# Reordered loads, scans and products and another cut of the last tile in a three-stage attention, channel-mix and convolution kernel

## The chip, the cores and the metric
One core of one Trainium2 chip. The metric is the time of one execution on the device in microseconds, as the median of several runs. TensorE (PE in the rows) multiplies, with its weight loads shown apart (PEld); VectorE (DVE), ScalarE (ACT) and GpSimd (POOL) do elementwise work; SP issues DMA transfers in the order of its program.

## The reference
Three layers follow each other, on 2 sequences of 768 positions with 8 heads of 64 features (512 in all).

```python
# 1: decayed linear attention, block by block (lam near 0.98 for each head)
intra = einsum('bhic,bhjc->bhij', qb, kb) * Dmask          # lam ** (i - j) for i >= j
out   = einsum('bhij,bhjd->bhid', intra, vb) + einsum('bhid,bhde->bhie', qb * lam_pow, kv_state)
kv_state = lam_block * kv_state + einsum('bhsd,bhse->bhde', kb * rev_pow, vb)
# 2: channel mix
xk = mu_k * x + (1 - mu_k) * x_prev ;  xr = mu_r * x + (1 - mu_r) * x_prev
k = maximum(xk @ w_k, 0) ;  v = k * k @ w_v ;  x = sigmoid(xr @ w_r) * v      # w_k 512x1024, w_v 1024x512
# 3: gated projection
gate = sigmoid(causal convolution of x with 5 taps per channel)
out = (gate * (x @ w_val)) @ w_out
```

## The kernel before
**Attention** runs over 12 chunks of 128 positions (6 for each sequence), heads in four pairs. For each chunk n, TensorE does `scores(n)` (keys against queries, fp32, into PSUM), `inter(n)` (state against the decayed queries qd), `attend(n)` (values against the weighted scores pT) and `update(n)` (values against the decayed keys kdec). VectorE does `weigh(n)`, scores times the decay matrix dec, and `new_state(n)`. GpSimd does `decay_k(n)` and `decay_q(n)`, which give kdec and qd. ScalarE does `fade(n)` (the state times one decay) and `evacuate_x(p)`, which copies the sums of a pair of chunks out of PSUM into x as soon as both are attended. Each engine has one list of work, written out by hand; a wait in it holds all that stands behind it. The order of TensorE is in lines 851 to 900, that of the others at the ends of their blocks.

**Decays.** dec (8 scans, line 592) and qdec (4 scans, line 598) are made on VectorE from `prm`, a 20 KB table that also holds the mixing and convolution parameters. ScalarE's queue loads prm (line 414); SP's queue loads all else, in the order of lines 225 to 246: qk (queries and keys, 512 KB a chunk) and kv (keys and values by position, 512 KB, or 256 KB where a chunk has no update), then w_k, w_r and w_v in pieces of 1024 columns. Eight input buffers; a load into a used one waits for the products that read it.

**Channel mix and projection** run over 3 tiles of 512 positions, with the features on partitions. A product with a weight is done in three passes of fp32r matmuls (`three_pass`, lines 692 to 698): high x high, low x high, high x low, where `high` is a rounded copy (ScalarE) and `low` the remainder (`low` on GpSimd, line 289, or on VectorE, line 537). `hidden(t, n)` is one of 8 products of 12 matmuls with w_k, `receptance(t, m)` one of 4 with w_r, `value(t, m)` one of 4 products of 24 matmuls with w_v. Piece i of w_k serves hidden n = 2i and 2i+1. ScalarE's `relu` and VectorE's `square` take each hidden result out of PSUM, `kk_high` and `kk_low` split it, and `value(t, 0)` waits for all eight low parts. `mix_part` (ScalarE), `mix` (VectorE), `mix_high` and `mix_low` make xk and xr from x; the ones for xr of tile 0 need x of attention's last pair, so `evacuate_x(5)`.

**The end.** `project(t, c)` gives 128 positions of output, `evacuate` copies them (line 406), SP stores them (line 257). The last one is done in two halves of 256 columns, each with its own copy (line 411) and store (line 262), so that the first half is stored while the second is multiplied.

Of the kernel before, what the change touches and what calls it, by code (L numbers as in the profile page):

```python
# [31 lines left out]
WARM = 8  # L32
PIECE = 1024
OUT_CH = NT * CT


LAM_A, LAM_B, MU, CONV = 0, H, H + PAIRS, H + PAIRS + 2 * KT
# [12 lines left out]
def build(nc, prm_in, qk_in, kv_in, w_k, w_v, w_r, w_val, w_out, out):  # L50
    with ExitStack() as ctx:
        def sem(name):
            return ctx.enter_context(nc.semaphore(name))
# [8 lines left out]
        def place(name, shape, at, dt=F32):  # L62
# [82 lines left out]
            sem(z) for z in "p_ready state_ready kdec_ready qd_ready faded_ready x_ready".split()]  # L145
        wk_hi, wk_lo, wr_hi, wr_lo, wv_hi, wv_lo, w2_hi, w2_lo = [
            sem(z) for z in "wk_hi wk_lo wr_hi wr_lo wv_hi wv_lo w2_hi w2_lo".split()]
        wk_lo_first = sem("wk_lo_first")
        (xk_part, xk_full, xk_hi, xk_lo, xr_part, xr_full, xr_hi, xr_lo) = [
            sem(z) for z in "xk_part xk_full xk_hi xk_lo xr_part xr_full xr_hi xr_lo".split()]  # L150
        h_done, r_done, v_done, val_done, proj_done = [
# [53 lines left out]
        @block.sync  # L205
        def _(sp):
            def free(n):

                if n >= IN_BUFS:
                    sp.wait_ge(att_done, n - IN_BUFS + 1)  # L210
                    sp.wait_ge(update_done, updates(n - IN_BUFS))

            def load_qk(n):
                free(n)
                sp.dma_start(qk[n % IN_BUFS][:, :, :], qk_in[n]).then_inc(qk_here[n % IN_BUFS], 16)

            def load_kv(n):
                free(n)
                first = 0 if has_update(n) else 1
                sp.dma_start(kv[n % IN_BUFS][:, first:, :], kv_in[n, :, first:, :]).then_inc(kv_here[n % IN_BUFS], 16)  # L220

            def load_weight(raw, src, i, done):
                sp.dma_start(raw[:, i * PIECE:(i + 1) * PIECE], src[:, i * PIECE:(i + 1) * PIECE]).then_inc(done[i], 16)

            load_qk(0)
            load_qk(1)
            load_kv(0)
            load_kv(1)
            for p in range(1, NP - 1):
                load_qk(2 * p)  # L230
                load_qk(2 * p + 1)
                load_kv(2 * p)
                load_kv(2 * p + 1)
            load_qk(NCH - 2)
            load_qk(NCH - 1)
            load_weight(wk_raw, w_k, 0, wk_here)
            load_kv(NCH - 2)
            load_kv(NCH - 1)
            for i in range(1, 4):
                load_weight(wk_raw, w_k, i, wk_here)  # L240
            for i in range(2):
                load_weight(wr_raw, w_r, i, wr_here)
            sp.wait_ge(att_done, IN_BUFS)
            sp.wait_ge(update_done, updates(IN_BUFS - 1))
            for i in range(4):
                load_weight(wv_raw, w_v, i, wv_here)

            sp.wait_ge(h_done, FT * NT)
            for i in range(4):
                src = w_val if i < 2 else w_out  # L250
                sp.dma_start(w2_raw[:, i * PIECE:(i + 1) * PIECE],
                             src[:, i % 2 * PIECE:(i % 2 + 1) * PIECE]).then_inc(w2_here[i], 16)

            for n in range(OUT_CH):
                if n < OUT_CH - 1:
                    sp.wait_ge(out_ready, n + 1)
                    sp.dma_start(out[n * CH:(n + 1) * CH, :], out_sb[n // CT][:, n % CT, :]).then_inc(stored, 16)
                else:
                    for half in range(2):
                        cols = slice(half * DM // 2, (half + 1) * DM // 2)  # L260
                        sp.wait_ge(out_ready, n + 1 + half)
                        sp.dma_start(out[n * CH:(n + 1) * CH, cols], out_sb[n // CT][:, n % CT, cols]).then_inc(stored, 16)
            sp.wait_ge(stored, 16 * (OUT_CH + 1))

        @block.gpsimd
        def _(pool):
# [30 lines left out]
                                    pattern=[[-1, P]], channel_multiplier=1).then_inc(ident_ok, 1)  # L297
            pool.wait_ge(dec_ok, H)
            decay_k(0)
            decay_k(1)  # L300
            pool.wait_ge(qdec_ok, PAIRS)
            decay_q(1)
            decay_q(2)
            decay_k(2)
            decay_k(3)
            decay_q(3)
            for p in range(2, NP):
# [1 line left out]
                decay_k(2 * p + 1)  # L309
                decay_q(2 * p)  # L310
                decay_q(2 * p + 1)
            for i in range(1, 4):
                low(wk, wk_raw, i, wk_hi, wk_lo)
            for i in range(2):
                low(wr, wr_raw, i, wr_hi, wr_lo)
# [4 lines left out]
        def _(act):  # L320
# [81 lines left out]
            def evacuate(t, c):  # L402
                n = CT * t + c
                if n < OUT_CH - 1:
                    act.wait_ge(proj_done, n + 1)
                    nc.scalar.copy(out_sb[t][:, c, :], ps[:, bank_of("proj", t, c), :]).then_inc(out_ready, 1)
                else:
                    for half in range(2):
                        cols = slice(half * DM // 2, (half + 1) * DM // 2)
                        act.wait_ge(proj_done, n + 1 + half)  # L410
                        nc.scalar.copy(out_sb[t][:, c, cols],  # L411
                                       ps[:, (bank_of("proj", t, c) + half) % 8, 0:DM // 2]).then_inc(out_ready, 1)

            act.dma_start(prm[:, :], prm_in).then_inc(prm_here, 16)
            act.wait_ge(warm_ok, 1)
            nc.scalar.activation(spare[:, :], warm[:, 0:1], ACT.Sigmoid)
            act.wait_ge(qdec_ok, PAIRS)
# [11 lines left out]
                mix_high(0, k, 0)  # L429
            fade(8)  # L430
            evacuate_x(3)
            fade(9)
            mix_high(0, 3, 0)
            fade(10)
            evacuate_x(4)
            for i in range(3):
                high(wk, wk_raw, i, wk_here, wk_hi)
            evacuate_x(5)
            high(wk, wk_raw, 3, wk_here, wk_hi)
# [58 lines left out]
        def _(dve):  # L498
# [93 lines left out]
                nc.vector.tensor_tensor_scan(dec[:, i, :], prm[:, LAM_A + i:LAM_A + i + 1].to_broadcast([P, CH]),  # L592
                                             ident[:, :], 0.0, ALU.mult, ALU.add).then_inc(dec_ok, 1)
            dve.wait_ge(dec_ok, H)
            weigh(0)
            dve.wait_ge(zero_ok, 1)
            for a in range(PAIRS):
                nc.vector.tensor_tensor_scan(qdec[:, a, :], prm[:, LAM_B + a:LAM_B + a + 1].to_broadcast([P, CH]),  # L598
                                             zeros[:, :], 1.0, ALU.mult, ALU.add).then_inc(qdec_ok, 1)
            nc.vector.tensor_scalar(om[:, :], prm[:, MU:MU + 2 * KT], -1.0, 1.0, ALU.mult, ALU.add).then_inc(om_ok, 1)  # L600

            dve.wait_ge(halo_ok, B)
# [10 lines left out]
            for p in range(2, NP):  # L613
                new_state(2 * p)
                if p + 1 < NP:
                    weigh(2 * p + 2)
                    weigh(2 * p + 3)
                new_state(2 * p + 1)
                if p == 2:
                    mix(0, 0, 0)  # L620
                    mix(0, 1, 0)
                    mix(0, 2, 0)
                if p == 3:
                    mix(0, 3, 0)
                    mix_low(0, 0, 0)
                    mix_low(0, 1, 0)
                if p == 4:
                    mix_low(0, 2, 0)
                    mix_low(0, 3, 0)
                if p == 5:  # L630
                    low(wk, wk_raw, 0, wk_hi, wk_lo_first)
            for k in range(KT):
                mix(0, k, 1)

# [54 lines left out]

        @block.tensor  # L690
        def _(pe):
            def three_pass(to, pairs):
                last = len(pairs) - 1
                for i, (left, right) in enumerate(pairs):
                    nc.tensor.matmul(to, left(0), right(0), start=(i == 0), stop=False)  # L695
                    nc.tensor.matmul(to, left(0), right(1), start=False, stop=False)  # L696
                    done = nc.tensor.matmul(to, left(1), right(0), start=False, stop=(i == last))  # L697
                return done
# [74 lines left out]
            def hidden(t, n):  # L773
                if n == 0:
                    pe.wait_ge(xk_lo, KT * (t + 1))
                    if t == 0:
                        pe.wait_ge(p_ready, 2 * NCH)
                if t == 0 and n == 0:
                    pe.wait_ge(wk_lo_first, 1)
                elif t == 0 and n % 2 == 0:  # L780
                    pe.wait_ge(wk_lo, n // 2)
                if t == 0 and n == 2:
                    pe.wait_ge(x_ready, NP - 1)
                if t == 0 and n == 4:
# [20 lines left out]
            def value(t, m):  # L805
                if m == 0:
                    pe.wait_ge(kk_lo, FT * (t + 1))
                    pe.wait_ge(wv_lo, 4)
                pe.wait_ge(sq_ready, FT * t + KT + m + 1)
                three_pass(ps[:, bank_of("mlp", t, FT + KT + m), :],  # L810
                           [(lambda z, f=f: wv[z][:, f * DM + m * P:f * DM + (m + 1) * P], lambda z, f=f: kk[z][:, f, :])
                            for f in range(FT)]).then_inc(v_done, 1)

            def val(t, m):
                if m == 0:
# [13 lines left out]
            def project(t, c):  # L829
# [10 lines left out]
                bank = bank_of("proj", t, c)  # L840
                halves = [(bank, 0, DM)]
                if CT * t + c == OUT_CH - 1:
                    halves = [(bank, 0, DM // 2), ((bank + 1) % 8, DM // 2, DM)]
                    pe.wait_ge(out_ready, CT + 1)
                for b, lo, hi in halves:
                    three_pass(ps[:, b, 0:hi - lo],
# [9 lines left out]
            attend(0)  # L856
            update(0)
            scores(2)
            update(1)
            inter(1)  # L860
            attend(1)
            scores(3)
            inter(2)
            attend(2)
# [7 lines left out]
            for p in range(2, NP):  # L872
# [2 lines left out]
                    scores(2 * p + 3)  # L875
                inter(2 * p)
                inter(2 * p + 1)
                attend(2 * p)
                attend(2 * p + 1)
                if p + 1 < NP:  # L880
                    update(2 * p + 2)
                    update(2 * p + 3)
            for t in range(NT):
                for n in range(FT):
                    hidden(t, n)
                for m in range(KT):
                    receptance(t, m)
                for m in range(KT):
                    value(t, m)
# [65 lines left out]
```

## Time and profile before

| what | us |
|---|---|
| median of 3 runs | 277.77 (277.58 to 279.51) |
| the profiled execution, its time | 278.59 |
| the profiled execution, span of its instructions | 276.5 |
| TensorE busy in that span | 268.1 |

The profile is of one execution. Its times are microseconds from the start of the span; L592 is line 592. A row of a timeline has the start, the length, engine, line and operation, output and inputs with their shapes, and how many instructions it merges; in brackets stands how long the engine had been idle before and what released it. Matmuls overlap: their own length (0.39 us for 512 columns) is longer than the distance from one start to the next, and the second is what a product costs. The rows that carry the argument stand in groups below.

### The profile page before, as it was taken

The numbers are of one execution on the slowest core, as the hardware profiler recorded it, in microseconds if no ns is written. First come the engines' busy times: TensorE is split into PE (matmuls) and PEld (weight loads), VectorE is DVE, ScalarE is ACT, GpSimd is POOL, SyncE is SP. The second block draws the span as 40 slices with busy tenths as digits, with TensorE's granted clock in tenths as the row PEclk, the third lists the DMA queues.
The fourth block names the chain that finished last, engine by engine and source line by source line (L and its number), as shares of the span: only waits on it lengthen the run. The fifth ranks groups of instructions, "written<-read, shape, count | busy, mean of one in ns | idle before, by whom it ended". The sixth has DMA issues, their size and how long they took to land.

```text
span 276.5 us, 4258 instructions
## 1 busy us (share of the span) xinstructions
PE 268.1 (97%) x1740; PEld 225.0 (81%) x1740; DVE 167.3 (60%) x248; ACT 125.3 (45%) x223; POOL 48.7 (18%) x35
## 2 busy tenths in 40 slices
PE   8599988999999999999999999999999999999996
PEld 7589977888888888888888888888888888888885
DVE  4956981899979113455886535337978599425000
ACT  2137668769477213457821143749217305412121
POOL 1677757916900000000000000000000000000000
PEclk9999999999999999999999999999999999999999
DMA  7999995000000000000000000350000000310323
GB/s 253 414 405 409 406 406 229 0 0 2 0 0 0 2 0 0 0 0 2 0 0 0 5 0 0 117 188 0 0 0 2 0 0 0 116 38 0 114 78 114
DMA packets 7506, 22.83 MB, mean 83 GB/s; under 512 B 960, under 2 KB 1216, under 8 KB 7488
## 3 DMA queue, kind: packets, MB, share of 16 engines
q1 hardware_dynamic: 7344, 22.55, 21.1%
q8 instruction: 14, 0.23, 0.3%
q10 hardware_dynamic: 144, 0.02, 0.0%
q14 instruction: 4, 0.03, 0.0%
HBM read 19.42 MB, written 3.15 MB: 82 GB/s over the span
## 4 chain that ended last, share of the span: by engine, by line
PE 94%; DVE 2%; issue 1%; ACT 0%
PE ps L696 28%; PE ps L695 28%; PE ps L697 28%; PE ps L763 4%; PE ps L711 3%; PE ps L750 2%; PE ps L728 1%; DVE qdec L598 1%; DVE pT L505 0%; DVE state L522 0%; ACT out_sb L411 0%; DVE state L519 0%; DVE om L600 0%
## 5 line engine op out<-in xcount | busy, mean ns | idle before, releaser
L695 PE MATMUL ps<-xk_h,wk_h 128*128 128x512 f32 x96 | 37.5, 390 | 0.0
L697 PE MATMUL ps<-xk_h,wk_l 128*128 128x512 f32 x96 | 37.4, 389 | 0.0
L695 PE MATMUL ps<-kk_h,wv_h 128*128 128x512 f32 x96 | 37.3, 389 | 0.0
L696 PE MATMUL ps<-kk_l,wv_h 128*128 128x512 f32 x96 | 37.3, 389 | 0.0
L697 PE MATMUL ps<-kk_h,wv_l 128*128 128x512 f32 x96 | 37.3, 389 | 0.0
L696 PE MATMUL ps<-xk_l,wk_h 128*128 128x512 f32 x96 | 37.3, 389 | 0.0
L568 DVE SCALAR_TENSOR_TENSOR gate<-x,prm,gate 128x512 f32<-128x512 f32 x48 | 32.6, 744 | 0.0
L544 DVE SCALAR_TENSOR_TENSOR kk_f<-ps,ring 128x512 f32<-128x512 f32 x24 | 16.5, 688 | 23.8 <-ACT ring L364 23.8
L381 ACT ACTIVATE gate<-x,prm 128x512 f32<-128x512 f32 x12 | 8.6, 724 | 38.9 <-DVE x L554 38.9
L364 ACT ACTIVATE ring<-ps 128x512 f32<-128x512 f32 x24 | 14.3, 596 | 26.0 <-PE ps L697 26.0
L549 DVE TENSOR_TENSOR kk_l<-kk_f,kk_h 128x512 fp32r<-128x512 f32 x24 | 21.2, 883 | 1.8 <-ACT kk_h L368 1.8
L695 PEld LDWEIGHTS ps<-xk_h,wk_h 128*128 128x128 f32 x96 | 18.0, 188 | 3.9 <-issue 0.2
L695 PEld LDWEIGHTS ps<-kk_h,wv_h 128*128 128x128 f32 x96 | 18.0, 188 | 3.8
L696 PEld LDWEIGHTS ps<-kk_l,wv_h 128*128 128x128 f32 x96 | 18.0, 188 | 3.8
L696 PEld LDWEIGHTS ps<-xk_l,wk_h 128*128 128x128 f32 x96 | 18.0, 188 | 3.7
L697 PEld LDWEIGHTS ps<-xk_h,wk_l 128*128 128x128 f32 x96 | 18.0, 188 | 3.7
L697 PEld LDWEIGHTS ps<-kk_h,wv_l 128*128 128x128 f32 x96 | 18.0, 188 | 3.7
L696 PE MATMUL ps<-w_l,gh 128*128 128x512 f32 (+1 forms) x52 | 19.4, 373 | 0.0
L697 PE MATMUL ps<-w_h,gl 128*128 128x512 f32 (+1 forms) x52 | 19.4, 373 | 0.0
L695 PE MATMUL ps<-w_h,gh 128*128 128x512 f32 (+1 forms) x52 | 19.4, 373 | 0.0
L695 PE MATMUL ps<-xr_h,wr_h 128*128 128x512 f32 x48 | 18.7, 389 | 0.0
L696 PE MATMUL ps<-xr_l,wr_h 128*128 128x512 f32 x48 | 18.7, 389 | 0.0
(72 smaller groups left out, 498.0 us busy)
## 6 DMA issues: line engine op xcount, KB each, us to landing
qk<-in_qk SPq DMA_DIRECT2D x12, 512.0 KB, 11.2
kv<-in_kv SPq DMA_DIRECT2D x10, 512.0 KB, 12.0
out<-out_sb SPq DMA_DIRECT2D x11, 256.0 KB, 2.0
wk_raw<-in_w_k SPq DMA_DIRECT2D x4, 512.0 KB, 12.8
wv_raw<-in_w_v SPq DMA_DIRECT2D x4, 512.0 KB, 11.0
wr_raw<-in_w_r SPq DMA_DIRECT2D x2, 512.0 KB, 14.9
w_raw<-in_w_val SPq DMA_DIRECT2D x2, 512.0 KB, 4.4
w_raw<-in_w_out SPq DMA_DIRECT2D x2, 512.0 KB, 6.8
```

Of the source, the lines that this page charges most:

```text
L364: nc.scalar.activation(ring[:, n % 4, :], ps[:, bank_of("mlp", t, n), :], ACT.Relu).then_inc(relu_ready, 1)
L381: nc.scalar.activation(like(t, gate[t][:, k, :]), x_cols(t, k, HALO), ACT.Copy, scale=prm[:, col:col + 1]).then_inc(tap0, 1)
L544: nc.vector.scalar_tensor_tensor(out=kk_f[:, n, :], in0=ps[:, bank_of("mlp", t, n), :], scalar=0.0, in1=ring[:, n % 4, :], op0=ALU.max, op ...
L549: nc.vector.tensor_tensor(kk[1][:, n, :], kk_f[:, n, :], f32(kk[0][:, n, :]), ALU.subtract).then_inc(kk_lo, 1)
L568: nc.vector.scalar_tensor_tensor(out=like(t, gate[t][:, k, :]), in0=x_cols(t, k, HALO - j), scalar=prm[:, col:col + 1], in1=like(t, gate[t ...
L598: nc.vector.tensor_tensor_scan(qdec[:, a, :], prm[:, LAM_B + a:LAM_B + a + 1].to_broadcast([P, CH]), zeros[:, :], 1.0, ALU.mult, ALU.add). ...
L695: nc.tensor.matmul(to, left(0), right(0), start=(i == 0), stop=False)
L696: nc.tensor.matmul(to, left(0), right(1), start=False, stop=False)
L697: done = nc.tensor.matmul(to, left(1), right(0), start=False, stop=(i == last))
L711: last = nc.tensor.matmul(ps_s[n % 2][row][:, cols], qk[i][rows_of(row), 1, cols], qk[i][rows_of(row), 0, cols], start=True, stop=True)
L750: last = nc.tensor.matmul(place_of(n, row, a), state[rows_of(row), n % 4, a * D:(a + 1) * D], qd[rows_of(row), n % 4, a * P:(a + 1) * P], ...
L763: last = nc.tensor.matmul(place_of(n, row, a), kv[i][:, 1, h * D:(h + 1) * D], pT[:, n % 4, row, a * P:(a + 1) * P], start=(opens(n, False ...
```

## The change
1. prm is loaded by SP, first in its queue, no longer by ScalarE. The first loads come as prm, qk 0, qk 1, kv 0, qk 2, kv 1, qk 3, kv 2, kv 3.
2. VectorE scans qdec before it weighs chunk 0. GpSimd decays queries 1 before keys 1. TensorE does update(1) after inter(1) and attend(1).
3. hidden(0, 0), the first product with w_k, is done in the last pair of chunks, between inter(11) and attend(10). For this ScalarE copies the high part of piece 0 of w_k behind evacuate_x(3), and GpSimd makes its low part; VectorE makes the low parts of pieces 1 and 2, GpSimd that of piece 3.
4. value(0, 0) waits for each piece of w_v where it first reads it, not for all four at its start.
5. The last output tile is cut at column 384 (384 and 128 columns) instead of 256.

```diff
+CUTS = (0, 384, DM)
@@ SP
+            sp.dma_start(prm[:, :], prm_in).then_inc(prm_here, 16)
             load_qk(0)
             load_qk(1)
             load_kv(0)
+            load_qk(2)
             load_kv(1)
-            for p in range(1, NP - 1):
+            load_qk(3)
+            load_kv(2)
+            load_kv(3)
+            for p in range(2, NP - 1):
...
-                        cols = slice(half * DM // 2, (half + 1) * DM // 2)
+                        cols = slice(CUTS[half], CUTS[half + 1])
@@ GpSimd
             decay_k(0)
-            decay_k(1)
             pool.wait_ge(qdec_ok, PAIRS)
             decay_q(1)
+            decay_k(1)
             decay_q(2)
...
-            for i in range(1, 4):
+            for i in (0, 3):
                 low(wk, wk_raw, i, wk_hi, wk_lo)
@@ ScalarE
-            act.dma_start(prm[:, :], prm_in).then_inc(prm_here, 16)
...
             evacuate_x(3)
+            high(wk, wk_raw, 0, wk_here, wk_hi)
             fade(9)
             mix_high(0, 3, 0)
             fade(10)
             evacuate_x(4)
-            for i in range(3):
+            for i in range(1, 3):
                 high(wk, wk_raw, i, wk_here, wk_hi)
@@ VectorE
             dve.wait_ge(dec_ok, H)
-            weigh(0)
             dve.wait_ge(zero_ok, 1)
             for a in range(PAIRS):
                 nc.vector.tensor_tensor_scan(qdec[:, a, :], ...).then_inc(qdec_ok, 1)
+            weigh(0)
...
                 if p == 5:
-                    low(wk, wk_raw, 0, wk_hi, wk_lo_first)
+                    low(wk, wk_raw, 1, wk_hi, wk_lo_mid)
+                    low(wk, wk_raw, 2, wk_hi, wk_lo_mid)
@@ TensorE
-                if t == 0 and n == 0:
-                    pe.wait_ge(wk_lo_first, 1)
-                elif t == 0 and n % 2 == 0:
-                    pe.wait_ge(wk_lo, n // 2)
+                if t == 0 and n in (0, 6):
+                    pe.wait_ge(wk_lo, n // 6 + 1)
+                if t == 0 and n in (2, 4):
+                    pe.wait_ge(wk_lo_mid, n // 2)
...
-                    pe.wait_ge(wv_lo, 4)
+                def piece_of_wv(f):
+                    if t == 0 and m == 0 and f % 2 == 0:
+                        pe.wait_ge(wv_lo, f // 2 + 1)
...
-                    halves = [(bank, 0, DM // 2), ((bank + 1) % 8, DM // 2, DM)]
+                    halves = [((bank + i) % 8, CUTS[i], CUTS[i + 1]) for i in range(2)]
...
             scores(2)
-            update(1)
             inter(1)
             attend(1)
+            update(1)
             scores(3)
...
                 inter(2 * p + 1)
+                if p + 1 == NP:
+                    hidden(0, 0)
                 attend(2 * p)
...
-                for n in range(FT):
+                for n in range(1 if t == 0 else 0, FT):
                     hidden(t, n)
```

## Rows read from the trace of the kernel before

**Rows 1.** The page: span, busy time, GB/s in 40 slices, the stores.

```profile
span 276.5 us, 4258 instructions
...
PE 268.1 (97%) x1740; PEld 225.0 (81%) x1740; DVE 167.3 (60%) x248; ACT 125.3 (45%) x223; POOL 48.7 (18%) x35
...
GB/s 253 414 405 409 406 406 229 0 0 2 0 0 0 2 0 0 0 0 2 0 0 0 5 0 0 117 188 0 0 0 2 0 0 0 116 38 0 114 78 114
...
out<-out_sb SPq DMA_DIRECT2D x11, 256.0 KB, 2.0
```

**Rows 2.** The chain that ended last: start, length, what.

```profile
13.04 0.67 PE ps L750 x16
...
17.63 1.99 PE ps L711 x32
...
36.92 0.69 issue
...
38.43 1.90 PE ps L763 x32
...
43.75 0.80 issue
...
45.15 0.42 PE ps L695
```

**Rows 3.** Stretches: length, busy time by engine, granted clock, DMA share, GB/s.

```profile
45.20:77.80 32.60, 32.60 (x144) 26.99 (x145) 28.01 (x27) 23.09 (x37) 22.39 (x9) 1.00 0.02 7
77.90:270.90 193.00, 193.00 (x853) 159.88 (x852) 107.19 (x162) 78.69 (x134) 0.00 (x0) 1.00 0.07 25
...
57.30:77.10 19.80, 19.80 (x89) 16.41 (x88) 19.75 (x22) 13.96 (x24) 11.41 (x4) 1.00 0.00 1
```

**Rows 4.** Transfers issued at 0.74, 5.54, 23.49, 274.46 us: size, us to landing.

```profile
qk<-in_qk SPq DMA_DIRECT2D x1, 512.0 KB, 3.4
...
qk<-in_qk SPq DMA_DIRECT2D x1, 512.0 KB, 11.9
...
kv<-in_kv SPq DMA_DIRECT2D x1, 512.0 KB, 11.4
...
out<-out_sb SPq DMA_DIRECT2D x1, 128.0 KB, 1.7
```

**Rows 5.** Timeline of VectorE, the scans.

```profile
4.31 2.63 DVE L592 TENSOR_TENSOR_SCAN dec<-prm,ident 128x128 f32<-128x128 f32 x8 [3.11 <-DMA prm<-in_prm]
...
8.18 2.94 DVE L598 TENSOR_TENSOR_SCAN qdec<-prm,zeros 128x128 f32<-128x128 f32 x4
```

**Rows 6.** Timeline of GpSimd.

```profile
7.97 2.24 POOL L273 TENSOR_TENSOR kdec<-kv,dec 128x512 f32<-128x512 f32 x2 [6.50 <-DMA kv<-in_kv]
...
36.33 2.50 POOL L285 TENSOR_TENSOR qd<-qk,qdec 128x512 f32<-128x512 f32 x2
...
48.15 2.41 POOL L292 TENSOR_TENSOR wk_l<-wk_raw,wk_h 128x1024 fp32r<-128x1024 f32 x1
50.51 2.86 POOL L292 TENSOR_TENSOR wr_l<-wr_raw,wr_h 128x1024 fp32r<-128x1024 f32 x1
```

**Rows 7.** Timeline of TensorE: the first product with w_v.

```profile
77.87 0.39 PE L695 MATMUL ps<-kk_h,wv_h 128*128 128x512 f32 x1
```

**Rows 8.** Timeline of VectorE, 49 to 77 us.

```profile
49.70 7.69 DVE L529 SCALAR_TENSOR_TENSOR xr_f<-x,om,xr_f 128x512 f32<-128x512 f32 x4 [6.11 <-ACT xr_f L352]
57.31 0.68 DVE L544 SCALAR_TENSOR_TENSOR kk_f<-ps,ring 128x512 f32<-128x512 f32 x1
...
76.38 0.68 DVE L549 TENSOR_TENSOR kk_l<-kk_f,kk_h 128x512 fp32r<-128x512 f32 x1
```

**Rows 9.** The end: TensorE's timeline, then ScalarE's copies.

```profile
272.30 0.28 PE L697 MATMUL ps<-w_h,gl 128*128 128x256 f32 x1
272.42 0.28 PE L695 MATMUL ps<-w_h,gh 128*128 128x256 f32 x1
...
271.19 0.59 ACT L406 COPY out_sb<-ps 128x512 f32<-128x512 f32 x1 [2.13 <-PE ps L697]
...
274.06 0.37 ACT L411 COPY out_sb<-ps 128x256 f32<-128x256 f32 x1 [1.06 <-PE ps L697]
```

More of the change, by code:

```diff
@@ L147, in build @@
             sem(z) for z in "wk_hi wk_lo wr_hi wr_lo wv_hi wv_lo w2_hi w2_lo".split()]
-        wk_lo_first = sem("wk_lo_first")
+        wk_lo_mid = sem("wk_lo_mid")
         (xk_part, xk_full, xk_hi, xk_lo, xr_part, xr_full, xr_hi, xr_lo) = [
@@ L408, in evacuate @@
                     for half in range(2):
-                        cols = slice(half * DM // 2, (half + 1) * DM // 2)
+                        cols = slice(CUTS[half], CUTS[half + 1])
                         act.wait_ge(proj_done, n + 1 + half)
                         nc.scalar.copy(out_sb[t][:, c, cols],
-                                       ps[:, (bank_of("proj", t, c) + half) % 8, 0:DM // 2]).then_inc(out_ready, 1)
-            act.dma_start(prm[:, :], prm_in).then_inc(prm_here, 16)
+                                       ps[:, (bank_of("proj", t, c) + half) % 8, 0:CUTS[half + 1] - CUTS[half]]).then_inc(out_ready, 1)
             act.wait_ge(warm_ok, 1)
@@ L691, in _, with three_pass @@
         def _(pe):
-            def three_pass(to, pairs):
+            def three_pass(to, pairs, ahead=None):
                 last = len(pairs) - 1
                 for i, (left, right) in enumerate(pairs):
+                    if ahead:
+                        ahead(i)
                     nc.tensor.matmul(to, left(0), right(0), start=(i == 0), stop=False)
@@ L811, in value @@
                            [(lambda z, f=f: wv[z][:, f * DM + m * P:f * DM + (m + 1) * P], lambda z, f=f: kk[z][:, f, :])
-                            for f in range(FT)]).then_inc(v_done, 1)
+                            for f in range(FT)], piece_of_wv).then_inc(v_done, 1)
             def val(t, m):
```

## Prediction
> **What bounds the kernel now.** I read the page first. TensorE is busy 97% of the span and the DMA engines are full only at the front [rows 1]. The chain that ended last [rows 2] says the same: TensorE from 12.9 us on, before it VectorE's qdec scans, then two gaps inside a run of products that wait for nothing the profile names ("issue", 0.69 and 0.80 us), and from 45.15 us nothing but three-pass products. The stretches [rows 3] settle how much can be won: between 45.2 and 77.8 us and between 77.9 and 270.9 us TensorE is busy for the whole of both, at the full granted clock (1.00, the 2.4 GHz level), and a product of 512 columns costs 193.0/853 = 0.227 us. So these 225.6 of the 276.5 us are fixed. The change can act in front of 45 us, at the seams of those stretches, and in the last tile. I take the front in four steps and then the tail.
>
> **Step 1, parameters first, loads and scans reordered.** Today VectorE waits for prm until 4.31 us, scans dec until 6.94, weighs chunk 0, and only then scans qdec: four scans in 2.94 us, beside GpSimd's decay of the keys; weighing of chunk 1 comes after them, at 11.3 us [rows 5]. First on SP's queue, prm has no data ahead of it. The bounds of its landing are today's 3.6 us after the issue (4.3) and the 1.7 us of the last store, the shortest transfer in the trace [rows 4]; I take 2.1, which is qk chunk 0's 3.4 us less the 1.3 us that 512 KB take at the 400 GB/s of the page [rows 1, 4]. Then dec is scanned from 2.9 to 5.5 us and qdec, with GpSimd idle, at dec's rate of 2.63/8 each, to 6.8 us. Weighing chunk 0 starts at about its old 6.97 us. The price: one issue of 0.4 us stands before all loads of the queue, and since the transfers run at 400 GB/s up to about 42 us [rows 1], every later landing moves by about 0.4 (0 to 0.45) us. GpSimd takes up kv of chunk 0 at 7.97 [rows 6]; with the shift at 8.35, so attend(0) starts near 8.45 and gains nothing. The next steps gain. An attend takes 0.95 us (half of 1.90), a chunk's scores 1.0, an inter 0.67 [rows 2], an update some 0.5. So update(0) ends near 10.0 and scores(2), whose queries now come a place earlier, near 11.1. GpSimd has qd(1) by 8.35 + 1.36 + 1.25 = 11.0 at the latest [rows 6], and new_state(0) is done while scores(2) run. inter(1) starts near 11.1 against 13.04; behind it attend, update, scores, inter, attend make 4.8 us: attend(2) ends near 16.0 against 17.63 [rows 2]. Of the queues passed: kv of chunk 1 comes one place later, some 2.6 us behind kv 0, at 10.9 us, and attend(1) wants it at 11.8; keys 1 are decayed after queries 1, by 12.3 us, and update(1) wants them at 12.7.
>
> **Step 2, what the loads leave of it.** scores(5) needs qk of chunk 5. It is issued at 5.54 and lands 11.9 us later, at 17.44 [rows 4]; with the shift, 17.86. One of the pair of scores takes 1.0 us, so the pair ends at 18.86 against 17.63 + 1.99 = 19.62 [rows 2]: of 1.6 us, 0.76 are left. Past that point the transfers have slack over what they feed, and TensorE would finish inter(11) at 42.07 - 0.76 = 41.3 us.
>
> **Step 3, hidden(0,0) ahead of attend(10).** It now needs the low part of piece 0 of w_k from GpSimd. GpSimd's list there is bound by a load: kv of chunk 10, issued at 23.49, lands at 34.9 [rows 4], with the shift 35.35. Then one kdec (1.36, until the first of two qd starts at 36.33 today) and the two qd (2.50) [rows 6] end at 39.2; the subtraction of 1024 columns took 2.41 us uncontended [rows 6], where VectorE has it today in half of that: 41.65. ScalarE's high part is no limit: piece 0 of w_k stands ahead of kv 10 in the queue. hidden(0,0) therefore starts at 41.75 (41.3 without the shift; 42.1 if nothing is won before; 42.5 with both losses). Its 12 products take 12 x 0.227 = 2.72 us. attend(10) and (11) then take 2.0 us, as the pair before them (1.90 [rows 2], and 0.1 for the handover), where they take 3.1 now: the gap of 0.80 us in them should go. I take it for late instructions, as nothing in the program is waited for there; they were in at 44.55 us [rows 2], and the new stream gets to the same place behind 2.7 us more of products, near 45.1 us.
> So the last attention product ends, and evacuate_x(5) starts, at e = 41.75 + 2.72 + 2.0 = 46.5 us, against 45.2 today. TensorE itself is ahead: hidden(0,1) starts at 46.4 against 45.15 [rows 2] + 2.72 = 47.87, a lead of 1.5 us.
>
> **Step 4, what that lead meets.** Putting the product first delays everything that needs the last x: ScalarE's evacuation, high(wk,3), high(wr), mix_part, then VectorE's four mixes and the squares. Today the mixes start at 49.70 and last 7.69 us for four, since each two-input operation of VectorE waits for the end of GpSimd's running subtraction (three of them end 0.55 us after one), and the first square starts at 57.31, 12.1 us after e [rows 6, 8]. From there VectorE does not rest (19.75 of 19.80 us [rows 3]) until kk_low(7), which starts at 76.38, takes 0.68 and ends at 77.06; value(0,0), which waits for it, starts at 77.87 [rows 7, 8]. Slack: 0.8 us. In the new order the first mix is due at e + 4.5, as today, and GpSimd's low(wk,3) runs from e + 2.05, its first low(wr) from e + 4.4 to 6.8, the second to e + 9.6; the mixes end at e + 11.4. The first square is at 57.9, 0.6 late; the twenty us behind it move along; kk_low(7) ends at 77.65 and value(0,0) starts at 77.7, where TensorE arrives already at 46.4 + 132 x 0.227 = 76.35. It waits 1.3 us. Of 1.5 us gained, 0.17 is left: **front -0.17 us** (-0.6 to +0.6). The moved subtractions (two on VectorE, 1.2 us each, between 41.6 and 44 us) lie in its idle time, 6.11 us before 49.70 [rows 8]. Waiting for w_v by pieces costs nothing: kk_low is the later one, and the fourth piece, ready near 76.6, is wanted 6 x 0.227 x 3 = 4 us after the start. Behind value(0,0) nothing else moves.
>
> **Step 5, the cut at 384.** Two times 12 products of 256 columns at 0.120 us each make 2.88 us now; 512 columns take 0.227 [rows 3, 9]. On the line through both, 384 columns take 0.173 and 128 take 0.066: 2.08 + 0.80, the same 2.88. What comes behind shrinks: the copy of 128 columns 0.26 instead of 0.37 (512 take 0.59) [rows 9], the store 1.55 instead of 1.7 (256 KB take 2.0 [rows 1, 4]): -0.26 us. But no fp32r product under 256 columns stands in the trace. Low bound 0.066 each. High bound: the products of plain fp32 with 128 columns come as two records each of which, two products side by side, takes 0.062 (32 in 1.99 us [rows 2]), so one alone takes 4 x 0.062 = 0.25; if a short fp32r product falls back to that, the part costs 12 x 0.18 = 2.2 more. Between them I take 0.12: no row shows full 128x128 weight loads closer than the 0.120 of the 256-column part [rows 9]. That is +0.64, less 0.26: **tail +0.38 us** (-0.26 to +1.95).
> The Trainium skill, page "TensorE: Matmul & The Clock Gate", section "LDWEIGHTS (loading the stationary operand)", gives columns over 1.2, 107 ns for 128 of them; by it the tail would be +0.23, and it speaks against the line and so against the cut. No row shows it apart from the 256-column pace.
>
> **Sum.** Profiled execution: span 276.5 us, time 278.59, 2.1 us lying around it, and 0.8 over the median 277.77. Span: 276.5 - 0.17 + 0.38 = 276.7. Against the median: 277.77 + 0.21 = 278.0 us.
>
> **Rivals.** (a) The lead is kept: kk_low(7) is not later, because the mixes meet no subtraction of GpSimd or evacuate_x(5) starts by 45.3. Then the front gives -1.5, with the tail's +0.38 276.6 us, with the line's -0.26 276.0. For it: GpSimd has one piece less to do behind e. Against: the mixes start where both low(wr) run. Chance 0.12. (b) Short products fall back to the fp32 pace: tail +1.95, 279.6 us, slower. It decides from 0.088 us per product on (12 x 0.022 = 0.26 eats what the shorter end gives). Chance 0.22. (c) The front loses: the fetch gap does not go, or loads shift more, and e is 47.3: every tenth behind 46.67 is a tenth lost at value(0,0), +0.6; with the tail 278.8 us. Chance 0.15. (d) The line holds at 128 columns: front -0.17, tail -0.26, 277.3 us: no difference that can be seen. Chance 0.16. (e) My forecast, 278.0: 0.35.
>
> **Numbers.** The range from 276.6 to 280.0 reaches from (a) to (b) with its front a little worse, and leaves out under 0.15. About 1% (2.8 us) is what a measurement of this kernel can tell from no change. Faster by that needs 275.0, below (a) with the best tail: 0.03. Slower by it needs 280.5, (b) and (c) together with something over: 0.05. Within 1%: 0.92.
>
> **What would show it.** Right: scans of qdec over by 7 us at about 0.33 each; inter(1) near 11.1; hidden(0,0) starting near 41.75 behind GpSimd's wk_l; no "issue" gap in the last attend; VectorE's first square near 57.9; a TensorE wait of 1 to 1.5 us on kk_l before the first product with w_v; everything behind it 0.2 us earlier than now; then 128-column products 0.12 apart. Wrong: no wait before that product (a), 0.2 or more between short products (b), e past 47 (c), or a wait at another seam, as at receptance(0,0) for xr_l, where I count 0.7 us of slack.

## The result: 2.3 us slower, and the profile after

| | kernel before | changed kernel |
|---|---|---|
| median, us | 278.38 (277.58 to 279.51, 6 runs) | 280.68 (280.08 to 282.3, 6 runs) |
| profiled execution: time, span | 278.59, 276.5 | 282.30, 280.5 |

The ratio of the times is 1.0093 (95% interval 1.0057 to 1.0128). It lies above my range, whose upper end was 280.0 us. The 277.77 that I started from came from three runs; over the 80 runs of the kernel before beside the experiments the medians were 278.25 to 278.62, so 0.6 us of the miss is the base.

First, the parts that went as the sum had them. VectorE's timeline after (start, length, instruction): prm is there at 2.56 us, dec is scanned at the old pace, and the four qdec scans take 1.37 us where they took 2.94 [rows 5].

```profile
2.56 2.63 DVE L598 TENSOR_TENSOR_SCAN dec<-prm,ident 128x128 f32<-128x128 f32 x8 [1.37 <-DMA prm<-in_prm]
5.23 1.37 DVE L603 TENSOR_TENSOR_SCAN qdec<-prm,zeros 128x128 f32<-128x128 f32 x4
```

TensorE's timeline after: inter(1) at 11.02 us (13.04 before [rows 2]), attend(2) over at 15.9 (17.6), then the queries of chunks 4 and 5 are waited for, and the "issue" gap near 37 us is there again.

```profile
11.02 0.67 PE L759 MATMUL ps<-qd,state 64*64 64x128 f32 x16
...
16.45 2.44 PE L720 MATMUL ps<-qk 64*128 64x128 f32 x32 [0.57 <-DMA qk<-in_qk]
...
37.44 0.81 PE L759 MATMUL ps<-qd,state 64*64 64x128 f32 x18 [0.72 <-issue]
```

Then the part that I had not seen. TensorE between inter(10) and the first products with w_k, same view. inter(11) waits 1.81 us for VectorE's new state, and behind it the products come 0.43 us apart, not 0.227.

```profile
40.54 0.67 PE L759 MATMUL ps<-qd,state 64*64 64x128 f32 x16
43.02 0.67 PE L759 MATMUL ps<-qd,state 64*64 64x128 f32 x16 [1.81 <-DVE state L528]
43.61 0.50 PE L704 MATMUL ps<-xk_h,wk_h 128*128 128x512 f32 x1
...
44.76 0.63 PE L704 MATMUL ps<-xk_h,wk_h 128*128 128x512 f32 x1
45.19 0.63 PE L705 MATMUL ps<-xk_l,wk_h 128*128 128x512 f32 x1
```

VectorE at that time, and GpSimd. Two mix_low of xk take 3.83 us (1.07 and 2.84); in the kernel before they took 1.55 (0.96 and 0.68). In both kernels the first ends 0.55 us behind GpSimd's last decay of queries (38.83 before [rows 6], 39.23 after). The second waits for GpSimd's subtraction of piece 0 of w_k, which runs from 39.19 to 41.99, and new_state(10), which is behind it in VectorE's list, comes at 42.46.

```profile
38.71 3.83 DVE L541 TENSOR_TENSOR xk_l<-xk_f,xk_h 128x512 fp32r<-128x512 f32 x2
42.46 0.41 DVE L528 TENSOR_TENSOR state<-faded,ps 128x256 f32<-128x256 f32 x1
...
39.19 2.80 POOL L298 TENSOR_TENSOR wk_l<-wk_raw,wk_h 128x1024 fp32r<-128x1024 f32 x1
```

The kernel before, where no subtraction runs beside them:

```profile
38.43 1.55 DVE L535 TENSOR_TENSOR xk_l<-xk_f,xk_h 128x512 fp32r<-128x512 f32 x2
```

The clock, in stretches of the same execution (length; busy time and count of PE, PEld, DVE, ACT, POOL; granted clock; DMA share; GB/s). TensorE had been busy 1.21 of 3.00 us at the 2.4 GHz level (1.00); in the stretch behind, the granted clock is 0.51, the 1.2 GHz level, for 3.4 us. The eight products of that stretch cost 0.43 - 0.227 us each more than before, about 1.6 us.

```profile
40.00:43.00 3.00, 1.21 (x36) 0.91 (x33) 3.00 (x3) 2.80 (x3) 1.99 (x1) 1.00 1.03 410
...
43.90:47.30 3.40, 3.40 (x9) 2.64 (x9) 1.24 (x2) 0.00 (x0) 0.00 (x0) 0.51 0.55 219
```

From there all is late. ScalarE's last copy of x starts at e = 50.18 (45.2 before), VectorE's last kk_low ends at 81.34, and TensorE waits for it before the first product with w_v, at 81.39 instead of 77.87 [rows 7, 8].

```profile
50.18 1.02 ACT L333 COPY x<-ps 128x1024 f32<-128x1024 f32 x1 [7.08 <-PE ps L772]
...
80.66 0.68 DVE L555 TENSOR_TENSOR kk_l<-kk_f,kk_h 128x512 fp32r<-128x512 f32 x1
...
81.39 0.50 PE L704 MATMUL ps<-kk_h,wv_h 128*128 128x512 f32 x1 [1.11 <-DVE kk_l L555]
```

Behind it nothing moves until the last tile: TensorE is busy all of the 192.6 us from 82.0 to 274.6. The end, on TensorE and ScalarE; the rows of before are [rows 9].

```profile
276.57 0.33 PE L706 MATMUL ps<-w_h,gl 128*128 128x384 f32 x1
...
277.81 0.28 PE L705 MATMUL ps<-w_l,gh 128*128 128x128 f32 x1
277.92 0.28 PE L706 MATMUL ps<-w_h,gl 128*128 128x128 f32 x1
...
278.24 0.27 ACT L417 COPY out_sb<-ps 128x128 f32<-128x128 f32 x1 [0.81 <-PE ps L706]
```

The twelve products of 384 columns take 2.11 us, 0.176 each; those of 128 columns are 0.111 apart. From the first product of the last tile to the end of the span it takes 280.5 - 274.64 = 5.86 us, against 276.5 - 270.99 = 5.51: +0.35.

The account of this profile is 3.52 us at the first product with w_v and 0.35 at the tail, 3.9 of the 4.0 us by which the spans differ. It is the slowest of the six executions of the changed kernel (282.3 us against a median of 280.68), so the first question of the experiments is what the others look like.

### The profile page after: what moved, and what is told of

It reads as the page before. It is cut to its first block, busy times and chain, and to the rows that moved or that the text cites. A ratio compares the mean times of both kernels' runs of the same rounds, so it can differ in the third digit from the quotient of the medians.

```text
span 280.5 us, 4258 instructions
## 1 busy us (share of the span) xinstructions
PE 271.9 (97%) x1740; PEld 227.5 (81%) x1740; DVE 169.5 (60%) x249; ACT 125.5 (45%) x223; POOL 46.0 (16%) x34
## 4 chain that ended last, share of the span: by engine, by line
PE 75%; DVE 14%; DMA 4%; issue 3%; SPq 2%; ACT 1%; ACTq 0%; DVEq 0%
PE ps L704 24%; PE ps L705 24%; PE ps L706 24%; DMA qk<-in_qk 4%; DVE kk_l L555 3%; DVE xr_f L535 2%; DVE pT L511 2%; DVE xk_f L535 2%; DVE kk_f L550 2%; PE ps L720 1%; PE ps L772 1%; DVE xr_l L541 1%; SPq L216 1%; SPq L221 1%; DVE state L528 1%
## 5 line engine op out<-in xcount | busy, mean ns | idle before, releaser
L704 PE MATMUL ps<-xk_h,wk_h 128*128 128x512 f32 x96 | 38.1, 397 | 0.0
L706 PE MATMUL ps<-xk_h,wk_l 128*128 128x512 f32 x96 | 38.1, 397 | 0.0
L705 PE MATMUL ps<-xk_l,wk_h 128*128 128x512 f32 x96 | 38.1, 396 | 0.0
L706 PE MATMUL ps<-w_h,gl 128*128 128x512 f32 (+2 forms) x52 | 19.6, 376 | 0.0
L705 PE MATMUL ps<-w_l,gh 128*128 128x512 f32 (+2 forms) x52 | 19.6, 376 | 0.0
L704 PE MATMUL ps<-w_h,gh 128*128 128x512 f32 (+2 forms) x52 | 19.5, 375 | 0.0
```

## The experiments

Ten runs were made, one of them of the changed kernel itself, each against the kernel before on the same chip: e1 to e4 on one chip, e5 to e8 on a second, e9 and e10 on a third. Differences are of medians, in us, with the interval of the ratio behind; across chips only differences from the kernel before are compared.

**Theory A**: GpSimd's subtraction of piece 0 holds VectorE's mix_low(0,3), that delays new_state(10) and inter(11), and the delay is carried by ScalarE's last copy of x into VectorE's chain. **B**: the early product alone costs the time, as it stands ahead of the last attention pair. **C**: the loads that now start later cost it.

**The changed kernel again (e7).** No edit.

> The changed kernel as it is, for another profile and more times on the same chip as the others. In the first profile the granted clock fell to 0.51 between 43.9 and 47.3 us, behind the wait of inter(11), and seven products came 0.43 us apart: about 1.5 us. Theory A1 (the clock falls in each execution): the same 0.51, last copy of x near 50.2 us, 282 us. Theory A2 (it falls in some): clock 1.0 in this profile, products 0.227 us apart, last copy near 48.6 us, first product with w_v near 79.8 (1.9 us later than in the kernel before), 280.4 us. Either way the first product with w_v starts at the last copy's start plus 31.2 us.

Measured: 280.27 us (6 runs, 280.21 to 280.67), +1.74 (1.0048 to 1.0091). The profile has the wait and not the low clock:

```profile
42.75 0.67 PE L759 MATMUL ps<-qd,state 64*64 64x128 f32 x16 [1.55 <-DVE state L528]
43.35 0.50 PE L704 MATMUL ps<-xk_h,wk_h 128*128 128x512 f32 x1
46.31 1.97 PE L772 MATMUL ps<-pT,kv 128*64 128x128 f32 x32
...
48.33 1.02 ACT L333 COPY x<-ps 128x1024 f32<-128x1024 f32 x1 [5.25 <-PE ps L772]
...
79.55 0.50 PE L704 MATMUL ps<-kk_h,wv_h 128*128 128x512 f32 x1 [1.13 <-DVE kk_l L555]
```

Theory A2 holds: the clock falls in some executions only. e = 48.33, and e + 31.2 = 79.53, where the first product with w_v starts at 79.55. This profile is near the median of its six: 79.55 - 77.87 = 1.68, and 0.35 for the tail.

**Order on VectorE (e1).** new_state(10) first, then mix_low(0,3).

```diff
                 if p == 4:
                     mix_low(0, 2, 0)
-                    mix_low(0, 3, 0)
...
                 new_state(2 * p)
+                if p == 5:
+                    mix_low(0, 3, 0)
```

> The changed kernel with one step moved on VectorE: mix_low(0,3), the last low part of xk, comes behind new_state(10) instead of ahead of it. Theory A (VectorE's two-input mix_low(0,3) is held by GpSimd's subtraction of piece 0, which delays new_state(10) and so inter(11)): the 1.8 us wait of inter(11) goes, inter(11) starts near 41.2 us, hidden(0,0) still waits for mix_low(0,3) until about 42.6; last copy of x out of attention at 47.3 us, 2.9 earlier than the 50.2 of the changed kernel's profile; time about 1.1 us above the kernel before (0.65 at value(0,0), 0.47 from the cut), so about 1.2 us below the changed kernel. Theory B (the early product itself costs the time by delaying the last attention pair, and the wait of inter(11) is harmless): as slow as the changed kernel, +2.3 us. Theory C (the late loads do it): as slow as the changed kernel.

Measured: 279.25, +0.63 (1.0011 to 1.0041). The chain of A goes at once: inter(11) waits for nothing (one row with inter(10)), hidden(0,0) starts at 41.92 instead of 43.35, the last copy at 46.90.

```profile
40.38 1.35 PE L760 MATMUL ps<-qd,state 64*64 64x128 f32 x32
41.92 0.50 PE L705 MATMUL ps<-xk_h,wk_h 128*128 128x512 f32 x1 [0.19 <-DVE xk_l L541]
...
46.90 1.02 ACT L333 COPY x<-ps 128x1024 f32<-128x1024 f32 x1 [3.96 <-PE ps L773]
...
78.13 0.50 PE L705 MATMUL ps<-kk_h,wv_h 128*128 128x512 f32 x1 [1.13 <-DVE kk_l L555]
```

B and C fall as sole causes: the product still stands ahead of the last attention pair and the loads are the same, and yet the interval of this run (0.3 to 1.1 us) lies below that of e7 (1.3 to 2.5). What is left, 0.63 us, is still above what my prediction had for the whole change (0.21), but its mechanism is there: e = 46.90 against my 46.5, a wait of 1.13 us for kk_l against my 1.3. mix_low(0,3), now behind new_state(10), is still held: it takes 1.03 us from 40.83 and ends 0.55 us behind the subtraction (41.31), but nothing of attention stands behind it.

**Piece 0 on VectorE (e2).** GpSimd makes the low parts of pieces 1 to 3, none before 42 us. TensorE's waits for the low parts go with them (not shown).

```diff
                     mix_low(0, 3, 0)
+                    low(wk, wk_raw, 0, wk_hi, wk_lo_mid)
...
-                    low(wk, wk_raw, 1, wk_hi, wk_lo_mid)
-                    low(wk, wk_raw, 2, wk_hi, wk_lo_mid)
```

> The changed kernel with the low part of piece 0 of w_k made on VectorE (1.22 us, between mix_low(0,3) and new_state(10)), pieces 1 to 3 on GpSimd, so GpSimd subtracts nothing before 42 us. Theory A: mix_low takes 2 x 0.7 instead of 3.83 us, new_state(10) near 41.2, inter(11) at 41.6, hidden(0,0) at 42.3, last copy of x at 47.0; +0.35 at value(0,0), +0.47 from the cut: 0.8 us above the kernel before. Theories B and C: +2.3 us, like the changed kernel.

Measured: 279.67, +1.05 (1.0021 to 1.0043). Without a subtraction beside them the two mix_low take 1.68 us, not 3.83, and inter(11) waits 0.23:

```profile
38.63 1.68 DVE L541 TENSOR_TENSOR xk_l<-xk_f,xk_h 128x512 fp32r<-128x512 f32 x2
40.22 1.21 DVE L546 TENSOR_TENSOR wk_l<-wk_raw,wk_h 128x1024 fp32r<-128x1024 f32 x1
...
41.91 0.67 PE L757 MATMUL ps<-qd,state 64*64 64x128 f32 x16 [0.23 <-DVE state L528]
```

This is the holding shown by itself: the same two instructions on the same engine in the same place, and the one thing that runs beside them no more is GpSimd's subtraction. e is 47.52 and the product with w_v starts at 78.74, +0.87 where the rule of e gives 78.72.

**The product back behind attention (e3).**

```diff
-                if p + 1 == NP:
-                    hidden(0, 0)
...
-                for n in range(1 if t == 0 else 0, FT):
+                for n in range(FT):
```

> The changed kernel with hidden(0,0) back behind the last attention products, all else as changed: the subtraction of piece 0 stays on GpSimd at 39.2 us. Theory A: inter(11) still waits 1.8 us for new_state(10), to 43.0; the last copy of x starts near 45.8 (46.5 if the gap of 0.8 us in the last attend comes back), hidden(0,0) at 45.7; about 0.5 us late at value(0,0) plus 0.47 from the cut: +1.0 us (to +1.7 with the gap). Theory B: no wait matters, +0.4. Theory C: +2.3.

Measured: 278.65, +0.03 (0.9994 to 1.0019). I expected +1.0 and was wrong: inter(11) still waits (0.99 us in this profile), but without the product in front, attention ends at 45.1 as in the kernel before. The wait takes the place of the gap: inter(11) ends 1.06 us later than in the kernel before, and the two attends behind it take 2.05 us instead of 3.16, as the gap of 0.80 us did not come back. The first product with w_v starts at 77.81 us, as in the kernel before.

```profile
42.46 0.67 PE L759 MATMUL ps<-qd,state 64*64 64x128 f32 x16 [0.99 <-DVE state L528]
43.06 2.05 PE L772 MATMUL ps<-pT,kv 128*64 128x128 f32 x32
45.04 0.50 PE L704 MATMUL ps<-xk_h,wk_h 128*128 128x512 f32 x1
...
45.15 1.01 ACT L333 COPY x<-ps 128x1024 f32<-128x1024 f32 x1 [1.79 <-PE ps L772]
```

So B has its share: the wait costs time only where 2.7 us of product stand between it and the last attention pair. Both are needed for the 1.7 us, the wait and the product ahead; the product without the wait is e1, 0.26 us late at value(0,0).

**Parts 1 and 2 alone (e4)**, on the kernel before (prm, loads, scans, queries 1 first, update(1) later).

> The kernel before with parts 1 and 2 of the change alone: prm first on SP, loads reordered, qdec scanned before weighing, queries 1 decayed first, update(1) behind attend(1). Theory A (and my step 2): scores(4) and (5) wait for their queries, the gap near 37 us swallows most of the rest, products with w_k start 0.2 to 0.7 us earlier: -0.2 us (-0.7 to 0). Theory C (late loads are what costs): slower, +0.4 us or more.

Measured: 278.86, +0.24 (0.9993 to 1.0022): no difference that can be told. C falls as the cause of 1.7 us; a few tenths lie within the interval. Its profile (278.11 us, the fastest of its twelve) has inter(1) at 10.77 us, 2.3 earlier than [rows 2], and the first product with w_k at 44.62, where the same view of the kernel before has 45.08. Of the 2.3 us, 0.98 are left behind the scores of chunk 5, which wait 0.76 us for their queries: inter(7) starts at 29.79 against 30.77. Two products into inter(7) TensorE stops for 0.42 us with nothing awaited, and behind it 0.2 is left (attend(6) at 31.23 against 31.45). That 0.2 passes the gap near 37 us, as long here (0.72) as there (0.69); the gap in the last attend is 0.27 shorter.

```profile
17.48 1.16 PE L715 MATMUL ps<-qk 64*128 64x128 f32 x16 [0.76 <-DMA qk<-in_qk]
...
29.79 0.43 PE L754 MATMUL ps<-qd,state 64*64 64x128 f32 x2
30.64 0.66 PE L754 MATMUL ps<-qd,state 64*64 64x128 f32 x14 [0.42 <-issue]
31.23 1.97 PE L767 MATMUL ps<-pT,kv 128*64 128x128 f32 x32
...
37.43 0.81 PE L754 MATMUL ps<-qd,state 64*64 64x128 f32 x18 [0.72 <-issue]
...
44.09 0.60 PE L767 MATMUL ps<-pT,kv 128*64 128x128 f32 x6 [0.53 <-issue]
```

The kernel before at inter(7), attend(6) and (7):

```profile
30.77 0.75 PE L750 MATMUL ps<-qd,state 64*64 64x128 f32 x16
31.45 1.97 PE L763 MATMUL ps<-pT,kv 128*64 128x128 f32 x32
```

**The cut alone, and the cut back (e5, e6).** The constant `CUTS` alone: (0, 384, DM) in the kernel before, (0, 256, DM) in the changed one.

> The kernel before with the last tile cut at 384 and nothing else. The changed kernel's trace has 128-column products 0.111 us apart against 0.066 on the line: 12 x 0.045 = 0.54 us more, less about 0.1 for a shorter last copy: +0.4 to +0.5 us (my tail, +0.38). If short products were free or only the trace of one execution showed it: -0.2 us.

Measured: 278.65, +0.12 (0.9989 to 1.0024). Too close to tell from nothing or from my +0.38.

> The changed kernel with the cut back at 256. Theory A (wait of inter(11), then all behind it): 0.4 to 0.5 us below the changed kernel, +1.6 to +1.9 us above the kernel before. If the tail were the main loss: no slower than the kernel before.

Measured: 279.98, +1.45 (1.0039 to 1.0078), 0.29 below e7 on the same chip. I had expected 0.4 to 0.5 for either. e5 alone cannot be told from nothing; the six executions of e6 (279.90 to 280.21) all lie at or below the six of e7 (280.21 to 280.67), so the cut does cost something, 0.3 us by these times and 0.35 by the traces.

**The mixes before the weights (e8).** e1 with the cut at 256, and on ScalarE:

```diff
             evacuate_x(5)
+            for k in range(KT):
+                mix_part(0, k, 1)
             high(wk, wk_raw, 3, wk_here, wk_hi)
             for i in range(2):
                 high(wr, wr_raw, i, wr_here, wr_hi)
-            for k in range(KT):
-                mix_part(0, k, 1)
```

> e1 (new_state(10) ahead of mix_low(0,3)) with the cut at 256, and on ScalarE the four mix_part of xr ahead of high(wk,3) and the two high(wr). If value(0,0) is late because the mixes start 4.5 us behind the last copy of x and then meet GpSimd's subtractions, the mixes now start 1.7 us behind it and take 4 x 0.65; the first square comes near the last copy plus 7 us instead of plus 11.4; TensorE no longer waits for kk_l and keeps its lead: first product with w_v near 76.8 us, -1.1 us against the kernel before. If that chain is not the cause, it stays at e1 less the cut's 0.5: +0.2 us.

Measured: 277.80, -0.73 (0.9972 to 1.0001). The mixes take 2.74 us for four, not the 7.69 of [rows 8], and TensorE waits for no engine before the product with w_v:

```profile
49.54 2.74 DVE L535 SCALAR_TENSOR_TENSOR xr_f<-x,om,xr_f 128x512 f32<-128x512 f32 x4 [3.99 <-ACT xr_f L358]
55.23 0.69 DVE L550 SCALAR_TENSOR_TENSOR kk_f<-ps,ring 128x512 f32<-128x512 f32 x1 [2.95 <-ACT ring L370]
...
77.57 0.39 PE L707 MATMUL ps<-xr_h,wr_l 128*128 128x512 f32 x1
77.83 0.50 PE L705 MATMUL ps<-kk_h,wv_h 128*128 128x512 f32 x1
```

The profiled execution is among the slower of its twelve (278.42; the fastest 277.54), with attention ending at 47.9 us, so its 77.83 does not show a gain. kk_low(7) ends at 77.78 there, only just in time. I had expected -1.1; the interval of the -0.73 just reaches no change, so the gain is likely and not shown. This profile also shows that moving mix_low(0,3) does not take the hold away: here mix_low(0,2) starts 0.13 us behind the subtraction and is held for 2.78 us, ahead of new_state(10). Nothing waits for that, as TensorE is a microsecond later than in e1.

```profile
38.88 2.36 POOL L298 TENSOR_TENSOR wk_l<-wk_raw,wk_h 128x1024 fp32r<-128x1024 f32 x1
39.01 2.78 DVE L541 TENSOR_TENSOR xk_l<-xk_f,xk_h 128x512 fp32r<-128x512 f32 x1
```

**The same step on the changed kernel and on the kernel before (e9, e10).**

> The changed kernel with one step moved: on ScalarE the four mix_part of xr ahead of high(wk,3) and the two high(wr). The wait of inter(11) for new_state(10) stays. If the time behind the last copy of x is VectorE's chain, the wait of 1.1 us for kk_l (1.5 from product to product) ahead of the first product with w_v goes and TensorE arrives there 29.9 us behind the end of attention, near 78.2 us instead of 79.55: 1.3 us below the changed kernel, about +0.4 us against the kernel before. If it is not, the time stays at +1.7 to +1.9.

Measured: 279.30, +1.05 (1.0019 to 1.0063), 0.7 less than e7's +1.74; the two intervals overlap. With the wait of inter(11) still there (0.73 us in this profile), e is 48.54, and the product with w_v starts at 78.50 without a wait, where e + 31.2 would be 79.74. I expected +0.4 against the kernel before; attention ended 0.2 us later than in e7, and two of its twelve executions had a granted clock of 0.993 and took 281.4 us, like the first profile of the changed kernel.

> The kernel before with the same step moved on ScalarE and nothing else. There TensorE sets the pace from 45 us on and waits for nothing; the earlier squares are only slack: 0 us (-0.1 to +0.1), first product with w_v near 77.8 us. If it gains as much as e8 does (0.7 us), the early product has no part in e8's gain.

Measured: 278.03, -0.22 (0.9966 to 1.0006). In its profile kk_low(7) ends 2.1 us before TensorE wants it (74.98 against 77.08), where it had 0.8 us in the kernel before. That is slack that nothing uses: about zero, as expected, though -0.22 cannot be told from a small gain. Against the kernel before on its own chip e8 gains 0.5 us more than this, but the intervals overlap; that e8 is the fastest kernel is likely, not shown.

## Why the prediction was wrong, point by point

**Bound, steps 1 and 2: right up to the scores of chunk 5.** prm landed 1.8 us after its issue against my 2.1, scans, inter(1) (11.0 against 11.1) and attend(2) (15.9 against 16.0) are as worked out, the loads gave most of it back at the queries of chunk 5 (the pair of scores ended at 18.89 against 18.86), and the shift of the loads was there: GpSimd took up kv 0 at 8.11 instead of 7.97 us, +0.14 where I took 0.4, and kv 10 at 35.70 instead of 34.97. Step 2 then took the remaining 0.76 us as kept, down to inter(11) at 41.3. Most of it went: in e4 0.98 us stand ahead of inter(7) and 0.2 behind it, and in the changed kernel 0.72 and 0.2 (scores of chunk 6 at 28.06 against 28.78, attend(6) at 31.24 against 31.45), as inter(7) stops or takes 1.21 us there. Where no state is waited for, inter(11) ends at 41.7 (e1) and 41.9 (e4).

**Step 3: the step that failed.** It put inter(11)'s end at 41.3 us and hidden(0,0) at 41.75. I followed GpSimd's list up to the subtraction and priced that as "uncontended", because I looked at who could slow GpSimd. The other direction was left out: behind mix_low(0,2), from 39.7 us on, VectorE stood at mix_low(0,3), an operation with two inputs, with new_state(10) behind it. I had named the rule for it one step later, for the mixes ("each two-input operation of VectorE waits for the end of GpSimd's running subtraction"), and did not apply it here. It measured 2.84 us for that one mix_low, 1.1 to 1.8 us of waiting at inter(11), hidden(0,0) at 43.35 (43.61 in the first profile) against 41.75: 1.6 us.
The Trainium skill, page "GPSIMD Engine Reference", section "Key points", says that GpSimd shares its SBUF interfaces with VectorE and contends with instructions that have two SBUF inputs. The trace agrees, and gives the size: 2.84 us where the same instruction takes 0.68 with GpSimd idle.

**The clock: not in the prediction.** Behind the wait, the granted clock fell to 0.51 in one profile of the changed kernel and was 1.00 in the other. Mean clocks of 0.993 and 0.994 mark three executions, of the changed kernel and e9, at 281.4 to 282.3 us, 1.6 to 2.1 us over their medians; none of the 80 runs of the kernel before is above 279.8. It explains the first profile and is not in the median. It does not explain all of the spread: one execution of the changed kernel took 281.65 us at a mean clock of 0.999, and why is open.

**Step 4: right, and it carried the error.** The last copy of x plus 31.2 us is the start of the first product with w_v in five profiles of kernels with the early product and the old order on ScalarE: 46.90 to 78.13 (e1), 47.52 to 78.74 (e2), 48.33 to 79.55 (e7), 48.39 to 79.61 (e6), 50.18 to 81.39 (changed). My text had 46.5 to 77.7. I wrote that every tenth behind e = 46.67 is lost whole; e7 has e = 48.33, so 1.66, and measured 1.68. Rival (c) was the right road, with a cause I did not have and less than half the size (e = 47.3, 0.63 us behind 46.67). Rival (a), a lead that is kept, is what e8 and e9 make of it.

**Step 5: right.** 0.111 us between products of 128 columns against my 0.12, tail +0.35 against +0.38. Rivals (b), 0.25 each, and (d), 0.066, are out. The Trainium skill, page "TensorE: Matmul & The Clock Gate", section "LDWEIGHTS (loading the stationary operand)", gives columns over 1.2 for a weight load, 107 ns for 128 columns. The trace agrees within 4 ns: the last tile's products of 128 columns, and the weight loads ahead of them, come 0.111 us apart.

**The sum.** With the usual profile: 1.68 at value(0,0) against -0.17, and 0.35 against 0.38, on a base of 278.4 to 278.5 instead of 277.77. The term that was mis-sized is the front. Something is given back outside the span: 1.79 us lie there on average in e7 against 2.04 in the kernel before, so 1.68 + 0.35 - 0.25 = 1.78, and 1.74 were measured. The first six executions of the changed kernel had 2.30; the 0.5 us between the two is within their intervals, and no profile of a usual one of those six is there to explain it.

## What to carry to other kernels
When work moves onto one of two engines that share a path, price both directions: how long it takes there, and which instruction of the other engine will stand at that place of its list, with what behind it. A product that is moved ahead to fill a wait delays all that stood before it in the list; find the longest chain behind the displaced work and its slack (0.8 us here) before counting the lead (1.5 us). And if a lead is then lost to a wait, shorten the chain that the wait comes from: moving four short operations ahead of three weight copies took that wait away in e8 and e9.

## What the runs showed of the hardware
- VectorE's instruction with two SBUF inputs does not run slower beside a GpSimd subtraction, it waits for the end of it: 2.84 us from 39.7 us until 0.55 us behind the subtraction's end at 41.99, 2.78 in e8, 1.03 in e1 where less of the subtraction is left, and 0.68 with GpSimd idle. The subtraction that takes up its work while VectorE runs such an instruction is longer in turn: 2.80 us beside mix_low(0,2), 2.41 without.
- TensorE's granted clock went from 1.00 to 0.51 in one of two profiles of the changed kernel, after a stretch in which it was busy 1.21 of 3.00 us, and came back after 3.4 us; in the other it was busy 1.45 of the same 3.00 us and the clock stayed at 1.00, as in e3, e6 and e9, which have the wait too. So whether it falls varies between executions. What decides it is open.
- The gap near 37 us, 0.7 us in each of these kernels, lies 14 matmuls behind the scores of the same pair, whether they end at 35.5 (e10) or 37.1 us (e8). The gap in the last attend (0.80, 0.53) is gone in every kernel with the early product or the wait of inter(11) in front of it. A third stop, of 0.17 to 0.42 us two matmuls into inter(7), shows in e2, e3, e4, e6 and e7 and takes most of the lead of the reordered start. I take all three for late instructions; no run here took the data transfers away from them to show it.
- 1.8 us (1.78 to 1.82) instead of 2.04 lie outside the span, on average, in the kernels where GpSimd has one instruction fewer (changed, e1, e3, e6, e7, e8, e9), 2.04 to 2.06 in e2, e4, e5 and e10 as in the kernel before. Why is not known.
